# A recurrent attention, gated MLP and expert attention kernel: unit 2's query and key products move from the tail of a batch into the next batch's first chunks

## What is computed

```python
def _attn_ref(q, k, v, a_re, a_im) -> np.ndarray:
    B, H, S, D = q.shape
    mag = np.sqrt(a_re * a_re + a_im * a_im)
    scale = np.minimum(mag, 0.999) / (mag + 1e-06)
    a_re_n, a_im_n = (a_re * scale, a_im * scale)
    ...
    for t in range(S):
        ar, ai = (a_re_n[:, :, t, :, None], a_im_n[:, :, t, :, None])
        new_re = ar * S_re - ai * S_im
        new_im = ar * S_im + ai * S_re
        kv = np.einsum('bhd,bhe->bhde', k[:, :, t], v[:, :, t])
        S_re, S_im = (new_re + kv, new_im)
        y[:, :, t] = np.einsum('bhd,bhde->bhe', q[:, :, t], S_re)

def _moe_ref(x, w_in, conv_w, w_out) -> np.ndarray:
    h = np.maximum(x @ w_in, 0.0)
    ...
    for k in range(K):
        conv_out += conv_w[k][None, None, :] * hp[:, k:k + S, :]
    gate = 1.0 / (1.0 + np.exp(-conv_out))
    return (h * gate @ w_out).astype(np.float32)

def _moe2_ref(x, w_gate, wq, wk, wv, wo) -> np.ndarray:
    ...
    logits = x @ w_gate
    topk = np.argpartition(-logits, K, axis=-1)[..., :K]
    ...
    for e in range(E):
        ...
        scores = scale * (q @ k.transpose(0, 2, 1))
        causal = np.triu(np.ones((S, S), dtype=bool), 1)
        scores = np.where(causal, -1000000000.0, scores)
        ...
        ye = a @ v @ wo[e]
        for kk in range(K):
            mask = topk[:, :, kk] == e
            out += mask[..., None] * w[:, :, kk:kk + 1] * ye
```

## Time and profile before

| | |
|---|---|
| median of three runs | 809.81 (809.47 to 810.85) |
| profiled execution | 810.85, its span 808.9 |
| TensorE busy | 688.4 (85%), granted clock 0.958 of full speed |
| DVE, ACT busy | 613.9 (76%), 396.5 (49%) |
| recurrent stage of batch 1, 274.99 to 330.88 | TensorE busy 47.94 of 55.89, clock 0.88 |
| recurrent stage of batch 2, 458.57 to 511.53 | TensorE busy 47.01 of 52.96, clock 0.90 |
| recurrent stage of batch 3, 636.65 to 679.77 | TensorE busy 42.19 of 43.12, clock 1.00 |
| from 299.0 to 305.0 | TensorE busy 5.92 of 6.00, clock 0.51 |

### The profile page before, as it was taken

One profiled execution on the slowest core, in us unless ns is written; L12 is line 12 of the kernel. 1 busy time (PEld: TensorE's weight loads), 2 busy tenths in 40 slices (PEclk: granted clock), 3 DMA queues, 4 the chain that ended last, 5 costly groups with the idle time before them and its releaser, 6 DMA issues.

```text
span 808.9 us, 13053 instructions
## 1 busy us (share of the span) xinstructions
PE 688.4 (85%) x5160; PEld 515.6 (64%) x5160; DVE 613.9 (76%) x1234; ACT 396.5 (49%) x723; POOL 0.2 (0%) x4
## 2 busy tenths in 40 slices
PE   0025737999999988999999898999999999999998
PEld 0024636876656676876656677876657788776575
DVE  4999996899888756799988766799888765541463
ACT  6503055533757644533757653533766424333465
POOL 0000000000000000000000000000000000000000
PEclk9999577999999987999999998999999999999999
DMA  8384452410028461410018561410026540000001
GB/s 326 163 233 118 119 143 55 156 40 0 1 72 226 135 177 41 156 40 1 0 59 228 150 173 41 158 39 1 0 79 184 152 112 10 0 1 1 0 22 40
DMA packets 95837, 73.84 MB, mean 91 GB/s; under 512 B 10912, under 2 KB 87968, under 8 KB 95136
## 3 DMA queue, kind: packets, MB, share of 16 engines
q1 hardware_dynamic: 95776, 73.01, 30.0%
HBM read 49.34 MB, written 23.65 MB: 90 GB/s over the span
## 4 chain that ended last, share of the span: by engine, by line
PE 46%; DVE 33%; DMA 10%; ACT 5%; issue 3%; SPq 3%; DVEq 0%; ACTq 0%
PE wide L1371 6%; DVE cv L1010 5%; PE wide L1342 5%; PE wide L1390 4%; PE wide L1267 4%; PE wide L1332 4%; DVE m L839 3%; DMA out_dram<-h 3%; PE wide L1425 3%; PE wide L1366 3%; DMA heads_dram<-araw 3%; PE bank L1441 2%; PE wide L1279 2%; DMA heads<-heads_dram 2%; DVE heads L1014 2%
## 5 line engine op out<-in xcount | busy, mean ns | idle before, releaser
L1332 PE MATMUL wide<-x_hi_lo,win_hi 128*128 128x384 f32 x384 | 109.0, 353 | 1.5 <-DVE x_hi_lo L972 1.5
L1342 PE MATMUL wide<-heads,wout 128*128 128x384 f32 x256 | 89.6, 493 | 5.8 <-DVE heads L1014 5.8
L1267 PE MATMUL wide<-heads 96*128 96x128 f32 x384 | 58.9, 317 | 26.0 <-DMA heads<-heads_dram 26.0
L1010 DVE SCALAR_TENSOR_TENSOR cv<-h,wconv,cv 128x768 f32<-128x768 f32 x64 | 64.8, 1013 | 12.9 <-ACT cv L595 11.1
L1267 PEld LDWEIGHTS wide<-heads 96*128 96x128 f32 x384 | 54.7, 226 | 31.0 <-DMA heads<-heads_dram 27.5
L1050 DVE TENSOR_REDUCE nmax<-wide 128x1 f32<-128x768 f32 (+2 forms) x96 | 55.2, 616 | 24.7 <-PE wide L1399 24.6
L1332 PEld LDWEIGHTS wide<-x_hi_lo,win_hi 128*128 128x128 f32 x384 | 69.9, 188 | 6.1 <-issue 3.4
L1342 PEld LDWEIGHTS wide<-heads,wout 128*128 128x128 f32 x256 | 46.9, 189 | 37.7 <-DVE heads L1014 11.7
L1254 PE MATMUL wide<-ident,heads 96*128 96x96 f32 x160 | 20.6, 284 | 55.9 <-DMA heads<-heads_dram 55.9
L1390 PE MATMUL wide<-attn 64*128 64x512 f32 (+3 forms) x256 | 65.0, 482 | 2.3 <-ACT attn L618 2.3
L590 ACT ACTIVATE h<-wide 128x384 f32<-128x384 f32 x64 | 29.8, 491 | 71.4 <-DVE heads L1014 40.2
(11 more groups left out here) (138 smaller groups left out, 1389.4 us busy)
## 6 DMA issues: line engine op xcount, KB each, us to landing
heads<-heads_dram SPq DMA_DIRECT2D x96, 192.0 KB, 3.6
araw<-a_in SPq DMA_DIRECT2D x12, 768.0 KB, 6.6
araw<-qk_in SPq DMA_DIRECT2D x12, 768.0 KB, 6.7
heads_dram<-m SPq DMA_DIRECT2D x24, 384.0 KB, 2.8
heads_dram<-araw SPq DMA_DIRECT2D x24, 384.0 KB, 3.2
v<-v_in SPq DMA_DIRECT2D x4, 1536.0 KB, 6.8
out_dram<-h SPq DMA_DIRECT2D x24, 192.0 KB, 4.2
wout<-w_out_t SPq DMA_DIRECT2D x1, 1536.0 KB, 12.0
```

The source lines that it names most:

```text
L1010: STT(cb, hb[:, tap:tap + S], wconv[:, mt, tap:tap + 1], cb, ALU.mult, ALU.add).then_inc(s_c, 1)
L1267: last = MM(low[2 + quad][:, hh * P:(hh + 1) * P], k_of(c, hd), q_of(c, hd), start=True, stop=True)
L1332: last = MM(low[u % 2][:, 0:NT], w[:, k, mt * P:(mt + 1) * P], xs[:, k, n * NT:(n + 1) * NT], start=(k == 0 and part == 0), stop=(k == KT ...
L1342: last = MM(mlp_bank[u][:, 0:NT], wout[:, mt, k * P:(k + 1) * P], hgate(mt)[:, n * NT:(n + 1) * NT], start=(mt == 0), stop=(mt == MT - 1))
```

## The change

`store_unit(b, 2)` moves in SP's queue from the end of `main(b - 1)`, ahead of the last output store, to behind `load_heads(b, 3)` in `main(b)`, and with it `load_a(b + 1, 2)`. On DVE `scale_qk(b, 2)` and the four `qk_product`s move from the tail of `main(b - 1)` into chunks 0 and 1 of `main(b)`. `gate_sumsq(b + 2, 1)` moves ahead to slot 11. The gate chain of unit 2 for the next batch moves with its load: `squares` from chunk 1 to 3, `gate_sumsq` from chunk 2 to 4, `magnitude`, `ln` and `guess` from chunk 2 to 4. Batch 0 has no batch ahead of it and keeps its order, but for `magnitude(1, 2)`, which goes behind `copy_x(0, 4)`. The number and sizes of all instructions stay the same.

```diff
--- before.py
+++ after.py
@@ -485,8 +485,9 @@
                 if b == 0:
                     load_a(1, 1)
                     move_decay(0, 2, 3, 5)
-                    store_unit(0, 2)
-                    load_a(1, 2)
+                store_unit(b, UNITS - 1)
+                if more:
+                    load_a(b + 1, UNITS - 1)
                 load_heads(b, 4)
                 load_heads(b, 5)
                 if more:
@@ -508,9 +509,6 @@
                 store_out(b, 1)
                 if more:
                     move_decay(b + 1, UNITS - 1, 0, NC - 1)
-                    store_unit(b + 1, UNITS - 1)
-                if b + 2 < B:
-                    load_a(b + 2, UNITS - 1)
                 store_out(b, 2)
                 for r in range(2):
                     sp.wait_ge(s_out[r], 16 * NC // 2 * (b + 1))
@@ -669,23 +667,15 @@
                         w_squares(0, 2)
                         w_ln(0, 2)
                         w_guess(0, 2)
-                    if b == 0 and c == 4:
-                        magnitude(1, 2)
                     copy_x(b, c)
-                    if b and more and c == 1:
+                    if more and c == 3:
                         squares(b + 1, UNITS - 1)
-                    if b and more and c == 2:
+                    if more and c == 4:
                         magnitude(b + 1, UNITS - 1)
                         exp_tables()
                         ln(b + 1, UNITS - 1)
                         guess(b + 1, UNITS - 1)
                     if b == 0:
-                        if c == 3:
-                            squares(1, 2)
-                        if c == 4:
-                            exp_tables()
-                            ln(1, 2)
-                            guess(1, 2)
                         if c in (0, 1):
                             squares(1, c)
                         if c == 2:
@@ -954,6 +944,11 @@
                 for x in (1, 0):
                     qk_product(b, u, part, x)
 
+            def last_unit(b, part, x):
+
+
+                qk_product(b, UNITS - 1, part, x)
+
             def mask(b, c):
                 for quad in range(2):
                     n = 2 * (NC * b + c) + quad
@@ -1069,19 +1064,24 @@
                 more = b + 1 < B
                 if b:
                     mask(b, 0)
+                    scale_qk(b, UNITS - 1)
+                    last_unit(b, 1, 1)
                     state_sum(b, 0)
                 else:
                     first_chunks()
                 for c in range(0 if b else 2, NC):
                     if c + 1 < NC:
                         mask(b, c + 1)
+                        if b and c == 0:
+                            last_unit(b, 1, 0)
                         state_step(b, c)
                     if c + 1 < GAINS:
                         state_sum(b, c + 1)
+                    if b and c == 0:
+                        last_unit(b, 0, 1)
+                        last_unit(b, 0, 0)
                     if c:
                         x_low(b, c - 1)
-                    if b and more and c == 2:
-                        gate_sumsq(b + 1, UNITS - 1)
                     if b == 0 and c == 2:
                         gate_sumsq(1, 0)
                         gate_sumsq(1, 1)
@@ -1093,6 +1093,8 @@
                         write_w(1, 0)
                     if b and more and 1 <= c < NC - 1:
                         (norm if c % 2 else write_w)(b + 1, (c - 1) // 2)
+                    if b and more and c == 4:
+                        gate_sumsq(b + 1, UNITS - 1)
                 x_low(b, NC - 1)
                 if more and b == 0:
                     norm(1, 1)
@@ -1160,15 +1162,8 @@
                             inverse_second(b + 1, 2)
                         if t == 10:
                             decay(b + 1, UNITS - 1, 0, NC - 1)
-                    if b + 2 < B and t == 9:
-                        gate_sumsq(b + 2, 0)
-                if more:
-                    scale_qk(b + 1, UNITS - 1)
-                    qk_products(b + 1, UNITS - 1, 1)
-                if b + 2 < B:
-                    gate_sumsq(b + 2, 1)
-                if more:
-                    qk_products(b + 1, UNITS - 1, 0)
+                    if b + 2 < B and t in (9, 11):
+                        gate_sumsq(b + 2, (t - 9) // 2)
 
             def first_chunks():
```

## The result

The changed kernel is slower: 828.99 us (median of four runs, 827.47 to 832.26), beside 809.64 for the kernel before on the same chip (four runs, 809.03 to 810.85). By the ratio that is 19.7 us, where the prediction had 12.4; 809.81 x 1.0243 = 829.5 lies just above its range, which ended at 829. The profiled execution of the change, whose trace is read here, took 823.65 (span 821.7) and so less than any of those four. Three executions of the kernel before, all in the first session of the experiments, lie more than 1.5% above the fastest of that session and are left out of the ratios and of what is said of the spread.

What follows compares the result with a forecast made beforehand. Waits for chunk 3's heads and copy_k, plus lower clock behind them, bound the recurrent stage. New holes gave batch 1 +3.1, batch 2 +6.0, batch 3 +3.3, batch 0 nothing: +12.4, so 822.2 us, range 812.5 to 829.

Steps and rivals of the forecast that it cites:

- the round trip: Chunk 4: unit 2's stores, gate load and heads arrive late; a hole of 4.1 in batches 1 and 2, 1.7 in batch 3.
- T4: Start of scores(b, 4), counted from z: 31.2 forecast in batches 1 and 2, 28.8 in batch 3; 27.07 undisturbed.
- the clock behind the hole: Matmuls after TensorE's idleness run at 1.2 instead of 2.4 GHz: 2.82 lost in batches 1 and 2, 1.6 in batch 3.
- Chunk 3: TensorE's waits for heads at scores(b, 3), 3.76 in batch 1 and 1.72 in batch 2, were to go.
- the products: Unit 2's products on DVE in chunks 0 and 1 cost nothing, as DVE waits there; uncovered, 0.91 per batch.
- the copies: TensorE's wait of 3.26 for ACT's copy_k at chunk 3 was to go, the gate chain having moved.
- z: The first matmul of a batch's scores(b, 0), from which all times of that batch are counted.
- T5: Start of scores(b, 5), counted from z: 40.8 forecast in batches 1 and 2; 33.87 undisturbed.
- The end of the stage: At h_products(b, 0, 1), batches 1 and 2: T5 + 15.35 instead of 9.25, ACT's gate chain preceding copy_x(b, 5); 2.82 of clock.
- Batch 0: Only magnitude(1, 2) moves behind one copy_x, where ACT waits for TensorE's next chunk: costed at 0.
- Rival 5: ACT's table switch takes 1.3 longer in its new place, in two batches: 824.8 us; chance 0.03, within the forecast's.
- Rival 3: DMA contention is worse: stores 1.4 later, gate load and heads the full 8.48: 829.4 us; chance 0.07.

Runs made afterwards that it cites:

- load_last: The changed kernel with the next gates' load moved behind the heads of chunks 4 and 5: 818.75 us, ratio 1.0175 to the kernel before.
- filled: The changed kernel with useless matmuls where TensorE stood idle, ahead of scores(b,4) and h_products(b,0,1), batches 1 and 2: 825.58 us, ratio 1.0189 to the kernel before.
- chain_only: The kernel before with only unit 2's gate chain on ACT and DVE moved from chunks 1 and 2 to 3 and 4: 812.14 us, ratio 1.0118.
- chain_split: The kernel before with unit 2's gate chain cut in two, copy_x(b,3) between magnitude and ln, batches 1 and 2: 800.83 us, ratio 0.9905.
- chain_late: The changed kernel with unit 2's magnitude, tables, ln and guess issued behind copy_x(b,5), batches 1 and 2: 828.04 us, ratio 1.0245 to the kernel before.
- out_first: The kernel before with the last output store issued ahead of unit 2's next gate load on SP: 799.10 us, ratio 0.9898.

## Why the prediction was wrong in size and right in kind

Slower for the reasons given: that was right. Two terms of the sum were too small, both of them at chunk 4 of batches 1 and 2: the time of the round trip (stores, gate load, heads), which put T4 at 31.2, and the clock behind the hole, taken as a fixed 2.82. In the traces other terms came out smaller and cover most of it, so that they show 14.2 where the sum had 12.4. The larger part of the miss, from 14.2 to 19.7, is in no trace; its cause stays open, and more on it stands below.

**Chunk 3, the products, the copies: right.** The hole at `scores(b, 3)` closed in both batches. The products on DVE cost nothing: `scores(1, 3)` starts at z + 20.26, and 656.91 − 636.65 = 20.26 is what the undisturbed batch 3 of before shows. The wait for `copy_k` went.

**Chunk 4: the right hole, too small.** This is the step that failed most. I had the stores done at z + 23.2. SP went on at z + 24.45 in batch 1 (+1.25), z + 23.73 in batch 2 and z + 24.01 in batch 3. There are two parts to this: in batch 1 the first store was issued at z + 16.17 instead of 15.55, because the issue of the heads took 2.49 instead of 1.9; and the stores needed 8.2 to 8.5 (8.15 to 8.8 over three profiles) beside the heads of chunk 3, where I had 6.26 and an allowance of 1.4. The 6.26 was the faster of two like cases in the trace that I had. In batch 2 of the kernel before the same four stores, with no heads of chunk 3 beside them, needed 469.09 − 461.29 = 7.80 (7.36 and 7.53 in its other profiles):

```profile
461.29 1.07 SPq L435 DMA_DIRECT2D heads_dram<-m  x2
...
469.09 0.55 SPq L404 DMA_DIRECT2D araw<-a_in  x1
```

It wasn't DVE that held the stores: the last product ended at 289.34 + 1.81 = 291.15, and the first store was issued at 292.24. Then gate load and heads: 9.33 and 8.46 (8.5 to 9.9 over three profiles) where I had 8.0, although batch 0's row said 8.48. I had shortened that without a row for it. T4 came at 33.8 and 32.9 (means of three) instead of 31.2: +2.6, of which the stores are 1.2 and gate load and heads 1.4, and +1.7, of which they are 0.7 and 1.0. `load_last` shows 3.4 and 3.1 of the hole as the gate load's, within the 1.5 named there. With T4 at 33.8 the change gained nothing at all in batch 1 by closing the first hole: T4 was 33.4 there before.

**The clock: right level, wrong firmness.** I took 2.82 as what a hole costs. The six stretches from T4 to T5 lost 2.1 to 5.9, 3.7 on average, so +0.8 for each. In batch 3, where I had put 1.6, it cost nothing in three profiles, and 5.9 in the filled kernel's. A single number for this term could not be right; the range should have carried it.

**The end of the stage: right.** T5 to the end was 15.0 (14.1 where T5 was late, since DVE then had a start) instead of 15.35. The wait ahead of `h_products(b, 0, 1)` was 3.22 in the batch shown and 4.8 in the five others, so the one of over 4; beside it stands one of 1.88 ahead of `outputs(b, 5)`, for DVE's `x_low` (0.58 where T5 was late), that I hadn't seen. Behind it the next z came 2.9 and 1.7 later, where I had 2.82 for both.

**Batch 0: not nothing.** I had put `magnitude(1, 2)` behind one `copy_x` at zero. In all three profiles of the change `h_products(0, 0, 1)` waits for 1.55, and the end comes 12.6 after T5:

```profile
145.96 0.42 PE L1327 MATMUL wide<-x_hi_lo,win_hi 128*128 128x384 f32 x1 [1.56 <-DVE x_hi_lo L967]
```

In `chain_only`, where batch 0 keeps its order and ran at the same clock, the wait is 0.39 and the end comes 11.46 after T5. The order of before in batch 0 was the one of `chain_split`, with a copy between `magnitude` and `ln`, and the change closed it up. The price is 1.2. In the means of three it doesn't show (+0.4 ahead of z of batch 1), because two of the profiles of before lost 1.5 by the clock there.

**The rule of the Trainium skill**, page "ScalarE: Activation LUTs", section "What ACT_TABLE_LOAD costs", has 1.38 for a drain beside the 1.28 of the load. In the chain above the load begins at 329.95 and lasts 1.28, and `ln` starts at 331.24: the measured switch is 1.28 and next to nothing more. The trace doesn't agree with the page's drain, and the measurement decides. Rival 5 is out.

**The sum against the traces.** Batch 1 +6.5 (forecast 3.1), batch 2 +5.3 (6.0), batch 3 +1.9 (3.3), ahead of them +0.4: 14.2 against 12.4. In batch 1 the terms are T4 +2.6, clock up to T5 +1.1, end of the stage −0.65, behind it +0.1, and 0.3 because the one profile of before that I started from had a slow batch 1. In batch 2 the first two are +1.7 and +0.6; against them stand −0.65 at the end of the stage, −1.1 behind it, and −1.1 because that same profile's batch 2 was faster than the mean of three. Rival 3 named the cause (stores later, gate load and heads the full 8.48); its own batch 3 term did not come.

**What the traces don't hold.** The ten executions of the change took 827.4 on average at a granted clock of 0.951; 24 of before in the later sessions 808.2 at 0.961. That is 19.2, and the profiled three of each differ by 14.2 (825.7 and 811.5). There are 5.0 between. The executions of the change without a trace ran at a lower clock than those with one (0.949 against 0.957, and 828.1 against 825.7), so that the mean of ten lies 1.7 above the profiled ones; before's profiled ones happen to lie 3.3 above its mean at nearly the same clock (0.959). Among before's 24 a clock lower by 0.01 goes with 4.0 us more. So a part of the 19.2 may be clock that the traces don't show. Whether the change lowers it by its holes or by chance stays open; `filled` (0.967 in its three other runs, with the same waits) speaks for the holes. It does not settle it.

What of the difference is waiting and what is clock can be summed from windows of 1 us (idle time, and busy time multiplied by what the granted clock lacks of full speed). From 60 us to the end, TensorE's idle time is 64.5, 68.0 and 70.4 in the profiles of before and 81.8, 81.0, 80.6 in those of the change, 13.5 more; the busy time lost to the clock is 25.7, 22.6, 18.8 and 22.0, 20.7, 21.4. So in the traces the change costs by waits: it moved the clock losses and took none away. In the filled kernel the same sum from 300 to 600 us is 1.7, against 12.3, 15.3 and 14.5 in the three of the change, which is where its 8.3 came from.

## What to carry to other kernels

A transfer that closes a round trip through memory (store, load back, use) is late by its whole chain: count from the release of the first store, not from the last, and take the slowest of the like cases that the trace has already, undiminished. Before moving a unit of work to get one transfer out of another's way, try the exchange of the two issues: here two lines gave a ratio of 0.990 where the large change gave 1.024. And where an engine has no slack in a stage, moving a block of 4 us there moves the hole; cutting the block at a place where the waiting copy can slip in took most of it away.

## What the runs showed of the hardware

- The length of a hole doesn't tell what the clock behind it costs. Holes of 2.46 and 3.27 had 12.73 behind them for a stretch of 6.8, one of 1.72 had 8.42, one of 1.91 and, in `chain_late`, one of 2.31 had 6.81. In one execution the holes of some 6.6 in two batches cost 2.7 and 5.9.
- Matmuls of no use in the wait kept the clock at 2.4 GHz: 6.81 from T4 to T5 in both batches, while the heads came as late as in the change.
- Four stores of 384 KB beside four loads of 192 KB needed 8.15 to 8.8 from the first issue to SP's going on (nine times in three profiles). Without those loads they needed 6.26 to 6.36 in batch 1 of before and 7.36 to 7.80 in batch 2, so what the loads add stays between 0.4 and 2.5. A load of 768 KB ahead of the heads delayed them by 3.1 to 3.4, in one profile.
- Thirteen executions of the kernel before on one chip spread from 803.28 to 814.42; the first had a granted clock of 0.966, the last one of 0.947, and by and large the longer ones have the lower clock. A difference of 1% needs many runs here: ten runs of `chain_split` gave an interval of 0.34% to either side, four of `out_first` one of 0.70%.
